# A three-part kernel (linear attention, a capacity-limited mixture of experts, a gated MLP): another order of an attention step, y in four array tiles, routing with 64-wide one-hots, and other places for pieces of the expert loop

## The chip, the cores and the metric

The kernel runs on one core of one Trainium2 chip. The metric is device microseconds (us) of one execution; lower is better. Two kernels are compared by the medians of several executions. The engines are TensorE (PE for its matmuls, PEld for its weight loads), VectorE (DVE), ScalarE (ACT), GpSimd (POOL), and SyncE (SP), which only issues DMAs here. Each engine runs its own instructions in the order written; engines meet through semaphores.

## What is computed

The reference chains three stages; the output of one is the input of the next (shapes: batch 4, 8 heads, 768 positions, head width 48; 3072 tokens of 384 values; 8 experts with 1024 hidden units; an MLP with 2048).

```python
def _attn_ref(r, k, v, w, u):
    for t in range(S):
        cur = np.einsum('bhd,bhe->bhde', u[None] * kt, vt)
        y[:, :, t] = np.einsum('bhd,bhde->bhe', rt, state + cur)
        state = wt[:, :, :, None] * state + np.einsum('bhd,bhe->bhde', kt, vt)

def _moe_ref(x, w_gate, w1, w2):
    # (token, expert) pairs by falling logit; an expert takes N // E tokens at most
    for e in range(E):
        h = np.maximum(x[mask] @ w1[e], 0.0)
        out[mask] = h @ w2[e]

def _moe2_ref(x, w_in, w_out):
    h = x @ w_in
    g = h * np.clip(h + 3.0, 0.0, 6.0) / 6.0
    return g @ w_out
```

## The kernel before

**Attention** (the function `attention`) works in 24 steps, one for each batch row `b` and chunk `c` of 128 positions, in the order n = 4c + b. A software pipeline (`pipelined`, line 43) lets every engine in its iteration m handle step m (`now`), step m-1 (`prev`) and step m-2 (`old`). The work of a step, by engine:
- DVE: scans of the decays (`fade`, L274, and `grow`, L285), `rt` (L281) and `kt` (L288) for step m; then `copy_predicated` (L295), which writes the masked scores of step m-1 over the parts of `aT` ahead of the diagonal and raises `masked`; then `total` (L302) of step m-2.
- PE: a transpose of the row of own terms (L422), the transposes of `kt` (L428), the projection `pick` (L408, heads packed and gate logits) of step m-2, the scores (L438) of step m, y from the state (L449) of step m-1, the row of own terms (L396) of step m+1, y from `aT` and `v` (L457) of step m-1, which raises `y_ready`, and the state's increment dS (L468). The scores wait for `masked` of step m-1, since they write the banks that L295 reads.
- ACT: the own terms' copy (L351), the diagonals of `aT` of step m, four activations for each half (`diagonal`, L333; the second half raises `diag_ready`), the copy of the transposed kt (L359), then the own row (L339), the copies of `pick`'s result (L374, L376), and `copy_xT` (L345) of step m-1, which waits for `y_ready`.

L295 of a step waits for `scores_ready` and `diag_ready` of that step. In each fourth step ACT and POOL also split a piece of `w_in` (L72, L78): every fp32 weight and activation of the later stages is held as a rounded part `_hi` and a remainder `_lo`, and each product is three matmuls (hi by hi, hi by lo, lo by hi; `product`, L1087).

**Routing** (DVE L834 to L945, PE L1047 to L1069) finds which expert fills first and which 384 tokens it takes: five rounds of threshold search (`cut`, `count`, `find_full`, `find_any`, `narrow`), then `candidates`, `locate`, `close`, `assign`, `name`. The ids of the tokens come from one-hots `at_q` of 128 columns (`name_q`, L938), multiplied on PE with small tables (`send_names`, L1069) and read by `take_ids` (L943 to L945). The first routing stands alone after attention; the one for expert e+1 runs inside the body of expert e.

**Experts** (`body` on each engine; e = 0 written out, 1 to 6 in a loop, 7 written out): 8 hidden tiles i of w1 and w2 (PE, with ACT L785 and DVE L989 between), the result `yT` split into hi (ACT L792) and lo (DVE L1001), then 16 tiles g of w_in and w_out, where between them stand a relu (ACT L799), the gate (DVE L1006), its rounding `act_hi` (ACT L804) and the remainder `act_lo` (POOL L735). PE computes tile g's `mid` (L1132 to L1137) and two tiles later its product with w_out. Constants (`OUT_AT_H`, `OUT_AT_G`, `NAME_AT`, `SPLIT_AT`, `SPLIT_OWN_AT` and so on) say after which i or g the pieces of routing, of splitting the next expert's weights (DVE L957) and of splitting w_out (POOL L713) are issued.

A separate block ahead of attention makes the identity matrix.

## Time and profile before

| | us |
|---|---|
| median of 3 runs | 865.16 |
| lowest, highest | 864.06, 865.38 |
| the profiled execution | 863.6 |
| its span (first to last instruction) | 861.9 |

Around the span lie 1.7 us. By engine the page gives PE 793.9 us busy (92% of the span), DVE 594.5, ACT 356.4, POOL 287.1. The span has these stages: attention until about 145 us, the first routing until 196, expert 0 until about 281, six loop bodies of 82.7 us each, and expert 7. In a row of a timeline the first number is the start, the second the length from the first start to the last modelled end; in brackets stand the idle time of the engine before it and what ended it. A matmul of 384 columns is recorded 0.33 us long while the next starts 0.17 to 0.18 us later, so where PE has waited, about 0.16 us must be added to the idle time in brackets to get what the wait cost.

### The profile page before, as it was taken

Reading aid. Unit: us, or ns where it says so; the run is one execution under the profiler, and the core shown is the slowest. Engines: PE = TensorE matmul, PEld = TensorE weight load, DVE = VectorE, ACT = ScalarE, POOL = GpSimd, SP = SyncE. Lnnn points to the kernel's source line nnn. Section 1 sums busy time; section 2 is a strip of 40 time slices with the busy share of each in tenths; the row PEclk is TensorE's granted clock in tenths of the full one; section 3 lists DMA queues with packets and bytes.
Section 4 is the critical chain, followed back from the end, with each engine's and each line's share of the span. In section 5 each row is a group of like instructions: output and inputs, shape, how many; then the busy total and the mean of one; then the engine's idle time right before and its main releaser. Section 6 shows DMA issues by size and latency. Waiting matters only on the chain.

```text
span 861.9 us, 17283 instructions
## 1 busy us (share of the span) xinstructions
PE 793.9 (92%) x6220; PEld 750.1 (87%) x6220; DVE 594.5 (69%) x1125; ACT 356.4 (41%) x783; POOL 287.1 (33%) x305
## 2 busy tenths in 40 slices
PE   5999998109999999999999999999999999999997
PEld 4999986109989999999999999999999999999996
DVE  7999997797698557665866676667667765863211
...
GB/s 299 200 246 240 213 241 56 0 125 123 74 50 115 38 0 73 100 27 0 90 93 18 21 93 86 0 49 76 76 0 49 100 52 0 49 102 51 1 1 27
DMA packets 22406, 70.13 MB, mean 81 GB/s; under 512 B 2912, under 2 KB 9312, under 8 KB 22368
## 3 DMA queue, kind: packets, MB, share of 16 engines
...
q0 software_dynamic: 3072, 9.44, 3.4%
q8 instruction: 24, 0.39, 0.2%
q14 instruction: 14, 0.11, 0.0%
...
## 4 chain that ended last, share of the span: by engine, by line
issue 40%; POOL 18%; PE 16%; DVE 5%; POOLq 2%; ACT 1%; DMA 0%; DVEq 0%; ACTq 0%
PE ps L1087 15%; POOL act_lo L735 14%; POOL out L749 3%; POOL rows L700 2%; DVE at_q L849 1%; POOLq L691 1%; DVE at_q L938 0%; DVE got L907 0%; DMA rows<-x_rows,gather_ids 0%; POOLq L734 0%; DVE cuts L846 0%; PE ps L1047 0%; ACT act_hi L804 0%; DVE w_lo L957 0%; DVE slot_add L910 0%
## 5 line engine op out<-in xcount | busy, mean ns | idle before, releaser
L735 POOL TENSOR_TENSOR act_lo<-gate,act_hi 128x384 fp32r<-128x384 f32 x128 | 146.2, 1143 | 364.5 <-ACT act_hi L804 364.0
L799 ACT ACTIVATE gate<-ps,three 128x384 f32<-128x384 f32 x128 | 74.5, 582 | 236.8 <-PE ps L1087 211.2
L1006 DVE SCALAR_TENSOR_TENSOR gate<-gate,ps 128x384 f32<-128x384 f32 x128 | 70.7, 552 | 103.1 <-ACT gate L799 100.4
L1087 PE MATMUL ps<-w_out_hi,act_hi 128*128 128x384 f32 x384 | 131.9, 344 | 6.9 <-POOL act_lo L735 6.0
L1087 PE MATMUL ps<-yT_hi,w_in_hi 128*128 128x384 f32 x384 | 132.7, 345 | 2.5 <-DVE yT_lo L1001 1.8
L1087 PE MATMUL ps<-yT_hi,w_in_lo 128*128 128x384 f32 x384 | 129.9, 338 | 0.0
L1087 PE MATMUL ps<-yT_lo,w_in_hi 128*128 128x384 f32 x384 | 129.5, 337 | 0.0
L1087 PE MATMUL ps<-w_out_hi,act_lo 128*128 128x384 f32 x384 | 128.7, 335 | 0.0
L1087 PE MATMUL ps<-w_out_lo,act_hi 128*128 128x384 f32 x384 | 128.4, 334 | 0.0
L785 ACT ACTIVATE act_hi<-ps 128x384 fp32r<-128x384 f32 x64 | 31.5, 492 | 141.8 <-PE ps L1087 140.8
L989 DVE SCALAR_TENSOR_TENSOR act_lo<-ps,act_hi 128x384 fp32r<-128x384 f32 x64 | 35.5, 555 | 77.6 <-ACT act_hi L785 77.6
L1087 PEld LDWEIGHTS ps<-w_out_hi,act_hi 128*128 128x128 f32 x384 | 72.1, 188 | 14.2 <-POOL act_lo L735 14.1
L1087 PEld LDWEIGHTS ps<-yT_hi,w_in_hi 128*128 128x128 f32 x384 | 72.1, 188 | 5.7 <-issue 4.1
L849 DVE TENSOR_TENSOR at_q<-value,cuts 128x768 bf16<-128x768 f32 x82 | 74.9, 955 | 1.4
L1087 PEld LDWEIGHTS ps<-w_out_lo,act_hi 128*128 128x128 f32 x384 | 72.1, 188 | 0.0
L1087 PEld LDWEIGHTS ps<-yT_lo,w_in_hi 128*128 128x128 f32 x384 | 72.1, 188 | 0.0
L1087 PEld LDWEIGHTS ps<-w_out_hi,act_lo 128*128 128x128 f32 x384 | 72.1, 188 | 0.0
L1087 PEld LDWEIGHTS ps<-yT_hi,w_in_lo 128*128 128x128 f32 x384 | 72.1, 188 | 0.0
L804 ACT ACTIVATE act_hi<-gate 128x384 fp32r<-128x384 f32 x128 | 66.2, 517 | 13.6 <-DVE gate L1006 13.6
L1087 PE MATMUL ps<-act_hi,w_hi 128*128 128x384 f32 x192 | 67.6, 352 | 0.0
L957 DVE TENSOR_TENSOR w_lo<-raw,w_hi 128x1024 fp32r<-128x1024 f32 x48 | 60.1, 1252 | 10.8 <-ACT w_hi L72 9.8
L72 ACT ACTIVATE w_hi<-raw 128x1024 fp32r<-128x1024 f32 x48 | 50.6, 1054 | 39.6 <-DMA raw<-in_w 39.6
...
## 6 DMA issues: line engine op xcount, KB each, us to landing
...
rows<-x_rows,gather_ids POOLq DMA_INDIRECT x24
out<-rows,scatter_ids POOLq DMA_INDIRECT x24
```

The lines of the kernel that those rows point to most:

```text
L72: act.activation(target[0][:, cols], self.raw[:, slot, :], ACT.Copy).then_inc(self.split_hi, 1)
L700: pool.indirect_dma_start(rows[:, t, :], None, x_dram, bass.IndirectOffsetOnAxis(gather_ids[:, t:t + 1], 0)).then_inc(moved, 16)
L735: pool.tensor_tensor(act[1][:, (H1 + g) % 3, :], gate[:, g % 2, :], act[0][:, (H1 + g) % 3, :].bitcast(F32), ALU.subtract).then_inc(g_lo, 1)
L749: pool.indirect_dma_start(out, bass.IndirectOffsetOnAxis(scatter_ids[:, t:t + 1], 0), rows[:, t, :], None).then_inc(moved, 16)
L785: act_.activation(act[0][:, i % 3, :], mid[i % 2], ACT.Relu).then_inc(act_hi, 1)
L799: act_.activation(gate[:, g % 2, :], mid[g % 2], ACT.Relu, bias=three[:, 0:1]).then_inc(gate_relu, 1)
L804: act_.activation(act[0][:, (H1 + g - 1) % 3, :], gate[:, (g - 1) % 2, :], ACT.Copy).then_inc(act_hi, 1)
L849: dve.tensor_tensor(above[:, half, :], value[:, half].unsqueeze(2).to_broadcast(shape), cuts[:, :].unsqueeze(1).to_broadcast(shape), ALU.i ...
L957: dve.tensor_tensor(target[1][:, cols], weights.raw[:, i % 2, :], target[0][:, cols].bitcast(F32), ALU.subtract).then_inc(expert_lo, 1)
L989: dve.scalar_tensor_tensor(act[1][:, i % 3, :], mid[i % 2], 0.0, act[0][:, i % 3, :].bitcast(F32), ALU.max, ALU.subtract).then_inc(h_lo, 1)
L1006: dve.scalar_tensor_tensor(gate[:, g % 2, :], gate[:, g % 2, :], 6.0, mid[g % 2], ALU.min, ALU.mult).then_inc(gate_ready, 1)
L1087: last = pe.matmul(out_, w, d, start=start and n == 0, stop=stop and n == len(passes) - 1)
```

## The change

- The first step's decays get a DMA of their own (`first_w`), ahead of the rest of `wrk`. The identity is made inside attention's block; the block ahead of it goes.
- y from the state goes to four 64 by 64 tiles of the array in place of two: for odd head pairs `a` the output halves are swapped (`half`), and even and odd pairs write different banks (3 and 4). `pick_gate` is permuted on the host to match, and `copy_xT` reads two banks. dS and the own row share bank 2 with the transposed kt, with waits on `ktT_copied` and `total_ready`; the own terms move to bank 4, with waits on `xT_ready` and `own_copied`.
- The order of a step changes on PE and ACT (below).
- The one-hots of `name_q` have 64 columns (`J`), `send_names` takes two tiles of tokens in a matmul (12 matmuls for 24), and `take_ids` adds the halves and writes the ids in four small operations.
- In the expert loop: `rounded` and `rest_of` order the first tile's nine matmuls so that the three that need a `_lo` activation come last; ACT issues `act_hi` of g = 0 ahead of the relu of g = 1; splits, names, gathers and the choice move by the constants; w_out's later splits on POOL are issued in halves.

PE, one full step in the steady part of attention. L438 and L444 are the scores, L449 before and L468 after are y from the state, L457 and L476 are y from `aT`. Before:

```order
L422 MATMUL attn_ps<-ident,attn_own_row 128x68
L428 MATMUL attn_ps<-ident,attn_kt 128x128 x4
L408 MATMUL attn_ps<-attn_pick_gate,attn_xT 128x104 x4
L438 MATMUL attn_ps<-attn_rt,attn_kt 128x128 x8
L449 MATMUL attn_ps<-attn_rt,attn_state 64x128 x8
L396 MATMUL attn_ps<-attn_rk,attn_u 64x128 x4
L457 MATMUL attn_ps<-attn_aT,attn_v 48x128 x8
L468 MATMUL attn_ps<-attn_v,attn_ktT 64x48 x8
```

PE, the same step after the change:

```order
L444 MATMUL attn_ps<-attn_rt,attn_kt 128x128 x8
L449 MATMUL attn_ps<-ident,attn_own_row 128x68
L454 MATMUL attn_ps<-ident,attn_kt 128x128 x4
L430 MATMUL attn_ps<-attn_pick_gate,attn_xT 128x104 x4
L468 MATMUL attn_ps<-attn_rt,attn_state 64x128 x8
L420 MATMUL attn_ps<-attn_rk,attn_u 64x128 x4
L476 MATMUL attn_ps<-attn_aT,attn_v 48x128 x8
L487 MATMUL attn_ps<-attn_v,attn_ktT 64x48 x8
```

The scores have moved from the fourth place to the first.

ACT, one full step in the same place, with the semaphores that each row waits for. Before:

```order
L351 ACTIVATE attn_own<-attn_ps 128x8 [waits attn_own_ready]
L333 ACTIVATE attn_aT<-ident,attn_own 128x128 [waits attn_y_ready,attn_own_copied]
L333 ACTIVATE attn_aT<-ident,attn_own 128x128 x3
L359 ACTIVATE attn_ktT<-attn_ps 128x512 [waits attn_dS_ready,attn_ktT_ready]
L333 ACTIVATE attn_aT<-ident,attn_own 128x128 x4
L339 ACTIVATE attn_own_row<-attn_ps 128x128 [waits attn_own_ready,attn_row_ready]
L374 ACTIVATE attn_x<-attn_ps 128x384 [waits attn_x_ready]
L376 ACTIVATE attn_logit_parts<-attn_ps 128x32
L345 ACTIVATE attn_xT<-attn_ps 128x512 [waits attn_y_ready]
```

ACT, the same step after the change:

```order
L367 ACTIVATE attn_own<-attn_ps 128x8 [waits attn_own_ready]
L372 ACTIVATE attn_ktT<-attn_ps 128x512 [waits attn_dS_ready,attn_ktT_ready]
L348 ACTIVATE attn_aT<-ident,attn_own 128x128 [waits attn_y_ready,attn_own_copied]
L348 ACTIVATE attn_aT<-ident,attn_own 128x128 x3
L354 ACTIVATE attn_own_row<-attn_ps 128x128 [waits attn_own_ready,attn_row_ready]
L387 ACTIVATE attn_x<-attn_ps 128x384 [waits attn_x_ready]
L389 ACTIVATE attn_logit_parts<-attn_ps 128x32
L361 ACTIVATE attn_xT<-attn_ps 128x2x2x128 [waits attn_y_ready]
L348 ACTIVATE attn_aT<-ident,attn_own 128x128 x4
```

The second half of the diagonals has moved from the fifth row to the last, behind the copy that waits for `y_ready`.

DVE, the first two hidden tiles of expert 0; `act_lo` is the remainder of a tile, `w_lo` a split of a weight piece, `rest` and `full_of` the verdict of a round (`find_full`). Before:

```order
L989 SCALAR_TENSOR_TENSOR act_lo<-ps,act_hi 128x384
L956 ISA
L957 TENSOR_TENSOR w_lo<-raw,w_hi 128x1024
L988 REGISTER_ALU
L989 SCALAR_TENSOR_TENSOR act_lo<-ps,act_hi 128x384
L854 ISA
L856 TENSOR_TENSOR rest<-need,ps 64x8
```

DVE, the same place after the change:

```order
L1028 SCALAR_TENSOR_TENSOR act_lo<-ps,act_hi 128x384
L1027 REGISTER_ALU
L1028 SCALAR_TENSOR_TENSOR act_lo<-ps,act_hi 128x384
L889 ISA
L891 TENSOR_TENSOR rest<-need,ps 64x8
```

The split has left the place between the two tiles.

The diff, cut to its core:

```diff
-        ktT_ps, y_ps, dS_ps, x_ps = ps[:, 2], ps[:, 3], bank(4, D), bank(5, PICK)
+        ktT_ps, dS_ps, x_ps = ps[:, 2], bank(2, D), bank(5, PICK)
+        own_row_ps = ps[:, 2].rearrange("p a t -> p (a t)")[:, PAIRS * D:PAIRS * D + PT]
+        y_ps = [ps[:, 3 + a % 2, a // 2, :] for a in range(PAIRS)]
+        y_by_bank = ps[:, 3:5, 0:PAIRS // 2, :]
+        own_ps = ps[:, 4, 2, 0:HP + H // 2]
+        own_at = ps[:, 4, 2, :].rearrange("p (g q) -> p g q", q=HP)[:, :, 0:H // 2]
...
-                    sp.dma_start(wrk[:, b, :], io["wrk"][n]).then_inc(wrk_in[b], 16)
+                    if n == 0:
+                        sp.dma_start(w[0], io["wrk"][0, :, 0:WF + 1]).then_inc(first_w, 16)
+                        sp.dma_start(wrk[:, 0, WF + 1:], io["wrk"][0, :, WF + 1:]).then_inc(wrk_in[0], 16)
+                    else:
+                        sp.dma_start(wrk[:, b, :], io["wrk"][n]).then_inc(wrk_in[b], 16)
...
-                    dve.wait_ge(wrk_in[b], 16 * (c + 1))
+                    if n == 0:
+                        dve.wait_ge(first_w, 16)
+                    else:
+                        dve.wait_ge(wrk_in[b], 16 * (c + 1))
...
-                act.activation(xT[:, b % 2], y_ps, ACT.Copy).then_inc(xT_ready, 1)
+                act.activation(xT[:, b % 2].rearrange("p (a k) t -> p k a t", k=2), y_by_bank, ACT.Copy).then_inc(xT_ready, 1)
...
                     n, b, c = now
                     act.wait_ge(own_ready, n + 1)
                     act.activation(own[:, b % 2].rearrange("p a h -> p (a h)").rearrange("p (g q) -> p g q", g=2),
-                                   own_at[c == CHUNKS - 1], ACT.Copy).then_inc(own_copied, 1)
-                    act.wait_ge(own_copied, n + 1)
-                    wait(act, y_ready, n - 1)
-                    diagonal(b, 0)
+                                   own_at, ACT.Copy).then_inc(own_copied, 1)
                     if c < CHUNKS - 1:
                         act.wait_ge(ktT_ready, n + 1)
                         wait(act, dS_ready, n - 1)
                         act.activation(ktT[:, b % 2], ktT_ps, ACT.Copy).then_inc(ktT_copied, 1)
-                    diagonal(b, 1).then_inc(diag_ready, 1)
-                    if b == 1:
-                        weights.hi(act, weights.w_in, bass.ds(c * PART, PART), c % 2, c // 2)
+                    act.wait_ge(own_copied, n + 1)
+                    wait(act, y_ready, n - 1)
+                    diagonal(b, 0)
                 if now and n + 1 < STEPS:
                     copy_row(n + 1)
...
                 if prev and now:
                     copy_xT(*prev)
+                if now:
+                    n, b, c = now
+                    diagonal(b, 1).then_inc(diag_ready, 1)
+                    if b == 1:
+                        weights.hi(act, weights.w_in, bass.ds(c * PART, PART), c % 2, c // 2)
...
+            def half(a, h):
+
+                return HP * (h if a % 2 == 0 else 1 - h)
...
+                wait(pe, ktT_copied, min(n, STEPS - B))
...
-                    pe.wait_ge(row_copied, n + 1)
-
-                    wait(pe, own_copied, n)
-                    if c < CHUNKS - 1:
-                        wait(pe, x_copied, n - 2)
-                    pe.transpose(own_ps[c == CHUNKS - 1], own_row[0:HP + H // 2, :], ident[0:HP + H // 2, 0:HP + H // 2]
-                                 ).then_inc(own_ready, 1)
                     pe.wait_ge(qk_ready, n + 1)
-                    if c < CHUNKS - 1:
-                        wait(pe, ktT_copied, n)
-                        for a in range(PAIRS):
-                            last = pe.transpose(ktT_ps[:, a, :], kt[:, b, a, :], ident[:, :])
-                        last.then_inc(ktT_ready, 1)
-                if old and (now or not prev):
-                    pick(old[0], old[1], now)
-                if now:
-                    n, b, c = now
                     wait(pe, masked, n)
                     for a in range(PAIRS):
                         for h in range(2):
                             part = slice(HP * h, HP * h + HP)
                             last = pe.matmul(ps[:, h, a, :], kt[part, b, a, :], rt[part, b, a, :], start=True, stop=True)
                     last.then_inc(scores_ready, 1)
-                    if n == 0:
-                        send_row(1)
+                    pe.wait_ge(row_copied, n + 1)
+                    wait(pe, own_copied, n)
+                    wait(pe, xT_ready, n - 1)
+                    pe.transpose(own_ps, own_row[0:HP + H // 2, :], ident[0:HP + H // 2, 0:HP + H // 2]).then_inc(own_ready, 1)
+                    if c < CHUNKS - 1:
+                        wait(pe, ktT_copied, n)
+                        wait(pe, total_ready, n - 1)
+                        for a in range(PAIRS):
+                            last = pe.transpose(ktT_ps[:, a, :], kt[:, b, a, :], ident[:, :])
+                        last.then_inc(ktT_ready, 1)
+                if old and (now or not prev):
+                    pick(old[0], old[1])
+                if now and now[0] == 0:
+                    send_row(1)
...
+                    pe.wait_ge(own_copied, min(n + 2, STEPS))
                     for a in range(PAIRS):
                         for h in range(2):
                             part = slice(HP * h, HP * h + HP)
-                            pe.matmul(y_ps[part, a, :], state[part, b, a, :], rt[part, b, a, :],
-                                      start=(a == 0), stop=True, skip_group_check=True)
+                            pe.matmul(y_ps[a][half(a, h):half(a, h) + HP, :], state[part, b, a, :], rt[part, b, a, :],
+                                      start=(a < 2), stop=True, skip_group_check=True)
                     if now:
                         send_row(n + 2)
                     pe.wait_ge(masked, n + 1)
                     pe.wait_ge(v_in[b], 16 * (c + 1))
...
-OUT_AT_H, OUT_AT_G = (3, 5, 6), (0, 1, 4)
-LOCATE_AT, NAME_AT, GATHER_AT, CHOOSE_AT, XT_AT = 4, 9, 9, 12, 16
+OUT_AT_H, OUT_AT_G = (5, 6, 7), (1, 3, 5)
+OUT_HALVES = {g + half: (len(OUT_AT_H) + i, half) for i, g in enumerate(OUT_AT_G) for half in range(2)}
+LOCATE_AT, NAME_AT, GATHER_AT, CHOOSE_AT, XT_AT = 4, 8, 8, 11, 16
 SPLIT_AT = (8, 10, 12, 14)
-SPLIT_OWN_AT = (0, 2)
+SPLIT_OWN_AT = (2, 4)
...
-                    q = MIDS * e + H1 + g
-                    if g < H2:
-                        act_.wait_ge(mid_ready, q + 1)
-                        if g >= 2:
-                            act_.wait_ge(g_lo, H2 * e + g - 1)
-                        act_.activation(gate[:, g % 2, :], mid[g % 2], ACT.Relu, bias=three[:, 0:1]).then_inc(gate_relu, 1)
+                    if g < H2 and g != 1:
+                        relu(g)
                     if g > 0:
                         act_.wait_ge(gate_ready, H2 * e + g)
                         if g > 3:
                             act_.wait_ge(g_used, (H2 - 1) * e + g - 3)
                         act_.activation(act[0][:, (H1 + g - 1) % 3, :], gate[:, (g - 1) % 2, :], ACT.Copy).then_inc(act_hi, 1)
+                    if g == 1:
+                        relu(1)
...
-                shape = [128, TILES // 2, 128]
-                dve.tensor_tensor(at_q[:, tiles, :], to_127[:, :].unsqueeze(1).to_broadcast(shape),
+                shape = [128, TILES // 2, J]
+                dve.tensor_tensor(at_q[:, tiles, :], to_63[:, :].unsqueeze(1).to_broadcast(shape),
...
-                link(dve.tensor_copy(ids_f[:, :], ids_ps[:, ET:2 * ET]))
-                dve.scalar_tensor_tensor(gather_ids[:, :], ids_ps[:, 0:ET], float(PT), ids_f[:, :], ALU.mult, ALU.add)
-                dve.scalar_tensor_tensor(new_ids[:, :], ids_ps[:, 0:ET], float(PT), ids_f[:, :],
-                                         ALU.mult, ALU.add).then_inc(ids_ready, 1)
+                link(dve.tensor_copy(odd_ids[:, :], ids_ps[J:2 * J, 2 * GROUPS:4 * GROUPS]))
+                link(dve.tensor_tensor(all_ids[:, :, :, :].rearrange("q c t h -> q (c t h)"), ids_ps[0:J, 0:2 * GROUPS],
+                                       odd_ids[:, :], ALU.add))
+                for ids in (gather_ids, new_ids):
+                    for h in range(2):
+                        last = dve.scalar_tensor_tensor(ids[h * J:h * J + J, :], all_ids[:, 0, :, h], float(PT),
+                                                        all_ids[:, 1, :, h], ALU.mult, ALU.add)
+                last.then_inc(ids_ready, 1)
...
-                    if g == NAME_AT - 2:
+                    if g == NAME_AT - 1:
                         name_q(e, 0)
-                    if g == NAME_AT - 1:
                         name_q(e, 1)
...
+            def rounded(out_, weight, data, start):
+
+                pe.matmul(out_, weight[0], data[0], start=start, stop=False)
+                pe.matmul(out_, weight[1], data[0], start=False, stop=False)
+
+            def rest_of(out_, weight, data, stop):
+
+                return pe.matmul(out_, weight[0], data[1], start=False, stop=stop)
...
+                        if i == 0:
+                            for k in range(KC):
+                                pe.wait_ge(xT_hi, 3 * e + k + 1)
+                                pe.wait_ge(expert_lo, 2 * LOADS * e + k + 1)
+                                rounded(mid[0], *of_w1(k), k == 0)
+                            for k in range(KC):
                                 pe.wait_ge(xT_lo, 3 * e + k + 1)
...
+    pick_gate[:, :, 1::2] = pick_gate[::-1, :, 1::2].copy()
```

## Rows read from the trace of the kernel before

**Rows 1.** Windows: busy us (count) of PE, PEld, DVE, ACT, POOL; clock; DMA

```profile
21.93:123.52 101.59, 101.51 (x1527) 91.93 (x1526) 96.74 (x127) 83.61 (x256) 43.87 (x47) 1.00 0.65 225
148.00:151.20 3.20, 0.76 (x4) 0.38 (x4) 2.23 (x14) 0.49 (x1) 0.00 (x0) 1.00 0.34 123
151.20:196.01 44.81, 8.15 (x101) 5.61 (x101) 36.73 (x92) 4.15 (x5) 4.08 (x4) 0.50 0.19 64
```

**Rows 2.** Timeline of PE over one attention step: start, us, what

```profile
71.21 0.28 PE L422 MATMUL attn_ps<-ident,attn_own_row 68*128 68x68 f32 x1
71.33 0.60 PE L428 MATMUL attn_ps<-ident,attn_kt 128*128 128x128 f32 x4
71.81 1.11 PE L408 MATMUL attn_ps<-attn_pick_gate,attn_xT 128*128 128x104 f32 x8
72.84 1.16 PE L438 MATMUL attn_ps<-attn_rt,attn_kt 64*128 64x128 f32 x16
73.94 1.09 PE L449 MATMUL attn_ps<-attn_rt,attn_state 64*64 64x128 f32 x16
74.96 0.66 PE L396 MATMUL attn_ps<-attn_rk,attn_u 128*64 128x128 f32 x8
75.44 1.04 PE L457 MATMUL attn_ps<-attn_aT,attn_v 128*48 128x128 f32 x16
76.32 0.62 PE L468 MATMUL attn_ps<-attn_v,attn_ktT 128*64 128x48 f32 x16
...
78.50 1.16 PE L438 MATMUL attn_ps<-attn_rt,attn_kt 64*128 64x128 f32 x16
```

**Rows 3.** Timeline of ACT and of DVE in the same step

```profile
72.92 0.58 ACT L359 ACTIVATE attn_ktT<-attn_ps 128x512 f32<-128x512 f32 x1
73.40 1.27 ACT L333 ACTIVATE attn_aT<-ident,attn_own 128x128 f32<-128x128 f32 x4
76.53 0.60 ACT L345 ACTIVATE attn_xT<-attn_ps 128x512 f32<-128x512 f32 x1
...
75.40 1.36 DVE L295 COPY_PREDICATED attn_aT<-attn_earlier,attn_ps 128x1024 f32<-128x1024 int32 x1
76.98 0.36 DVE L302 TENSOR_TENSOR attn_total<-attn_ps,attn_state 128x192 f32<-128x192 f32 x1 [0.22 <-PE attn_ps L468]
```

**Rows 4.** Timeline of PE at the start and the end of attention

```profile
8.40 1.12 PE L396 MATMUL attn_ps<-attn_rk,attn_u 128*64 128x128 f32 x8 [8.40 <-DMA attn_pick_gate<-in_pick_gate]
...
11.44 2.08 PE L438 MATMUL attn_ps<-attn_rt,attn_kt 64*128 64x128 f32 x16
...
15.93 0.38 PE L438 MATMUL attn_ps<-attn_rt,attn_kt 64*128 64x128 f32 x2 [0.25 <-DVE attn_aT L295]
...
139.81 1.16 PE L438 MATMUL attn_ps<-attn_rt,attn_kt 64*128 64x128 f32 x16
...
144.81 1.08 PE L457 MATMUL attn_ps<-attn_aT,attn_v 128*48 128x128 f32 x16
```

**Rows 5.** Timeline of DVE at the end of the first routing

```profile
181.97 3.43 DVE L938 TENSOR_TENSOR at_q<-to,q_f 128x1536 bf16<-128x1536 bf16 x2
```

**Rows 6.** Timeline of PE: where it waited in the expert bodies

```profile
250.33 0.44 PE L1087 MATMUL ps<-yT_hi,w_in_hi 128*128 128x384 f32 x1 [0.79 <-DVE gate L1006]
310.52 0.42 PE L1087 MATMUL ps<-yT_hi,w_in_hi 128*128 128x384 f32 x1 [0.22 <-DVE yT_lo L1001]
316.06 0.44 PE L1087 MATMUL ps<-w_out_hi,act_hi 128*128 128x384 f32 x1 [0.21 <-POOL act_lo L735]
340.27 0.76 PE L1069 MATMUL ps<-names,at_q 128*128 128x6 bf16 x24
361.82 0.44 PE L1087 MATMUL ps<-w_out_hi,act_hi 128*128 128x384 f32 x1 [0.39 <-POOL act_lo L735]
370.61 0.18 PE L1055 MATMUL ps<-full,ones 128*128 128x1 bf16 x1 [0.28 <-DVE full L858]
809.39 0.44 PE L1087 MATMUL ps<-w_out_hi,act_hi 128*128 128x384 f32 x1 [0.58 <-POOL act_lo L735]
```

112 lines of the change are left out of this document (66 added, 46 removed).

## The prediction

> **What bounds the kernel now.** I read the windows first, then the timeline of one attention step engine by engine, then the edges of attention, then the places where PE waited in the expert bodies. The first window runs from the scores of step 2 to those of step 20: 18 steps in 101.59 us, 5.64 us each, PE marked busy in all of it, DVE in 96.74 of it [rows 1]. In the timeline of PE the groups of a step follow each other without a wait, and the next step's scores start 5.66 us after the last ones (72.84 to 78.50) [rows 2]. DVE has 0.22 us a step in which it waits for PE's dS [rows 3]. So attention is bound by PE's own work, with DVE close behind. In the experts PE is bound too; what can be had there are its few waits [rows 6].
>
> **The order of an attention step.** This is the part that decides. Follow the semaphores after the change. The scores of step m+1 wait for `masked` of step m. That is the predicated copy on DVE, which waits for `diag_ready` of step m. The second half of the diagonals, which raises it, now stands behind `copy_xT` of step m-1 on ACT, and ACT issues in order. `copy_xT` waits for `y_ready` of step m-1, and y from `aT` of step m-1 is issued by PE in the same iteration as the scores of step m, and behind them. That closes a circle: scores, then nearly all of PE's step, then ACT, then DVE, then the next scores. Before, the diagonals needed only the own terms (PE's first group); they ended at 74.67 and the copy started at 75.40, so they were never late [rows 3].
>
> What one turn of the circle costs, from the starts of successive groups [rows 2]: scores 1.10 us (73.94 - 72.84, the change of array tiling at its end included), own terms 0.12, transposes of kt 0.48, `pick` 1.03, y from the state 0.60 (below), own row 0.48, y from `aT` to its end 1.04: together 4.85. Then ACT starts `copy_xT` 0.05 us after y's end (76.48 to 76.53); the next activation starts about 0.50 after that (after the 0.58 us copy it took 0.48); four diagonals 1.27; about 0.03 to DVE; the predicated copy 1.36; 0.05 back to PE [rows 3]. That is 3.26. One turn takes 8.11 us, against 5.66: 2.45 us more a step. PE's dS, DVE's scans (all of DVE's step is under 5.4 us) and POOL's work lie beside it and cost nothing.
>
> y from the state: eight matmuls are 16 records, two at a time in two diagonal tiles, in 1.02 us (73.94 to 74.96) [rows 2], some 0.11 us a pair and 0.2 for the change of tiling. With four tiles at once half of the steps of 0.11 go: 1.02 - 4 x 0.11 = 0.58, and I take 0.60. That four run at once no row shows. The upper bound is no gain, 1.02; a loss is excluded, since only the halves of odd pairs move. I take 0.60 because y from `aT` shows two column tiles over the same rows with different data (16 records in 76.32 - 75.44 = 0.88) and the scores show two row tiles: both directions are there.
>
> That row also answers a rule. The Trainium skill ("TensorE: Matmul & The Clock Gate", Part 3, The mechanism) says that weight loads overlap with running matmuls only where the row groups differ. By it even and odd pairs, on the same rows, would take turns, and y would stay at 1.02. The y from `aT` just quoted runs two at a time on one row group, which speaks against it.
>
> Summed over attention:
> - Steps 2 to 19, 18 turns: 18 x 2.45 = +44.1.
> - The last three turns have no transposes of kt: 8.11 - 0.48 = 7.63. The stretch from 123.52 [rows 1] to 139.81 [rows 4] is 16.29 us for three, 5.43 each. +6.6.
> - Turn 1 has no `pick`: 8.11 - 1.03 = 7.08, against 6.00 (15.93 [rows 4] to 21.93 [rows 1]). +1.1.
> - After the last scores: now the last y from `aT` starts 5.00 us later (139.81 to 144.81) [rows 4]; then it needs the whole turn, 7.63. +2.6. DVE's early choice of experts stands ahead of the last predicated copy and fits into its wait.
> - The start. Without the block of its own, and with the first DMA a little ahead, PE's first group, which waits for `pick_gate`'s DMA at 8.40 [rows 4], comes about 1.0 us sooner (a bound from below of 0; the queue is the same). The scores of step 0 then start at about 8.5 and not 11.44, but PE and the circle at the slow clock (scores 2.0, transposes 1.0, own row 1.1 behind the kt copy of 0.6, then 0.3 + 1.27 + 1.36 and handoffs) put step 1's at about 16.5 against 15.93 [rows 4]. +0.6, between -1.5 and +2.
>
> Together +55.0 us.
>
> **The routing that stands alone.** Two one-hot operations take 3.43 us at 128 columns [rows 5]; half as wide, 1.7 less 0.1: -1.6. The names of six groups and not three, one more linked operation and two more small ones in `take_ids` give back about 0.6. -1.0. The first tile's `rounded` part starts before the remainders of xT: -0.3. Sum -1.3.
>
> **The expert bodies.** To the bracketed idle times 0.16 us is to be added [rows 6].
> - The verdict of a round comes late in tile 1 because a split stands ahead of it on DVE: 0.28 + 0.16 = 0.44. With the split two tiles on, where DVE has room (there was one after tile 2 before), this goes. Seven bodies: -3.1.
> - Between the hidden tiles and w_in PE waits 0.22 + 0.16 for the remainder of y; at the first w_out tile 0.21 + 0.16 for POOL. The new order of the nine matmuls removes the first and the earlier `act_hi` most of the second, but DVE still has a cut ahead of the first gate, so the two give 0.41 together, not 0.75. Seven bodies -2.9. The last body has no cut: 0.38 + 0.74 = -1.1.
> - Names: 24 small matmuls in 0.76 us; half of them less, 0.3. -2.1.
> - Behind the transposes PE waits 0.39 for a remainder that POOL makes while DVE works off a cut and a split; the cut now stands one tile earlier. Half of it, -1.3.
> - In body 0 a late gate costs 0.79 + 0.16, behind DVE operations that POOL's long splits slow; halves and other places: -1.0.
>
> Sum -11.5, between -5 and -16; the lower end if POOL's gathers meet the same tiles as before and `take_ids`, which is longer, delays a gate.
>
> **Sum.** 863.6 + 55.0 - 1.3 - 11.5 = 905.8 for the profiled execution. The median of before lies 1.6 above its profiled execution, so 907.4; I say 907.
>
> **The rivals.**
> - *Pairs stay pairs.* The y from the state remains at 1.02. Then a turn is 8.53, and 0.42 x 23 = 9.7 us more: 917. For it: no row has four tiles; against it: y from `aT`. This is also what the rule above gives.
> - *The clock falls.* Each turn leaves PE without work from dS's end to the next scores: dS ends 5.4 us into a turn of 8.11, so 2.7 us. Before, the clock was at 1.00 (2.4 GHz) through attention, and went to 0.50 (1.2 GHz) at 151.2, behind 3.20 us in which PE was busy for 0.76 [rows 1]. If it fell in the turns, PE's 4.85 would near the pace of step 0 (scores 2.0 for 1.1) and grow by about 4.3: held down half of the time, +2.1 x 22 = 47, so 954. Against it: PE is busy for two thirds of a turn, and between 8.40 and 15.93, with waits between the groups, it came up (scores 2.08 long in step 0, 1.16 later) [rows 2, 4]. The Trainium skill (the same page, Part 1) has the clock halved by idleness and released by activity; the rows bear that out, and they leave open what two thirds would do.
> - *Faster than before.* The circle is not what binds: ACT gets past `copy_xT` in time. The place is ACT's queue between the row's copy and the diagonals. It decides at one point: with 3.26 us behind y's end, PE's stretch from the scores to that end must be under 2.4 us for the step to stay at 5.66, and it is 4.85 with every group in its written place. If the circle fell away, DVE would set about 5.36 us a step: -0.3 x 22 = -6.6, and 865.2 - 6.6 - 12.8 = 846. Only a misread order would give this.
> - *The bodies turn worse.* The gathers, the longer `take_ids` and two ACT splits in the last hidden tiles of body 0 cost as much as they free: -11.5 becomes 0, 919.
>
> **How the numbers follow.** Main case (four tiles, clock up, the bodies gain 5 to 16) 0.63, 900 to 915; pairs 0.14; bodies without gain 0.08; clock 0.09; no circle 0.05; 0.01 for a tie. The range 896 to 922 takes in the first three (about 0.85, less the tails) and leaves out the clock and the other side. Within 0.2% is about what a measurement can tell from no change. Faster 0.05, same 0.01, slower 0.94.
>
> **What would show it.** In the timeline of the changed kernel the scores come every 8.1 us; the predicated copy waits about 2.7 us a step for ACT's diagonals, and the diagonals follow `copy_xT` at once; PE's scores wait for the predicated copy. y from the state takes 0.6 us to the next group (pairs: 1.0). The clock stays at 1.00 until after attention. Attention ends near 200 us. In a loop body the waits for `full`, `yT_lo` and the first `act_lo` are gone and its length is near 81.4 us, not 82.7. I am wrong if the scores come every 5.4 us, if the clock column shows 0.50 inside attention, or if the diagonals start before y's end.

## The result: slower, and by more than forecast

The changed kernel takes 935.85 us (median of 4 runs, 933.97 to 938.06), the kernel before 864.61 us in the same comparison (863.86 to 865.38). The ratio is 1.0829, with a 95% interval of 1.0815 to 1.0843. The forecast was 907, with a range of 896 to 922: the direction was right, the size was not. The profiled execution of the changed kernel took 933.97 us, with a span of 932.2; that of before had a span of 861.9. All stage times below are from these two.

The page of the changed kernel: the span, PE's busy tenths and the clock in 40 slices, and two groups of attention (busy us, mean ns | idle before, releaser).

```profile
span 932.2 us, 17153 instructions
...
PE   5676766666219989999999999999999999999997
...
PEclk8888888897559989999999999999999999999999
...
L444 PE MATMUL attn_ps<-attn_rt,attn_kt 64*128 64x128 f32 x384 | 33.4, 320 | 68.1 <-DVE attn_aT L309 68.1
L309 DVE COPY_PREDICATED attn_aT<-attn_earlier,attn_ps 128x1024 f32<-128x1024 int32 x24 | 31.2, 1299 | 92.2 <-ACT attn_aT L348 92.2
```

Two things are new. PE waits 68.1 us before the scores (L444) for DVE's predicated copy (L309), and that copy waits 92.2 us for ACT's diagonals (L348). And the clock's row stands at 8, not 9, through the first eight slices, up to 186 us; attention ends near 230.

Now one attention turn on PE; compare [rows 2]. Start, us, what, and in brackets the idle time before it and who ended it.

```profile
119.15 1.16 PE L444 MATMUL attn_ps<-attn_rt,attn_kt 64*128 64x128 f32 x16 [2.90 <-DVE attn_aT L309]
120.24 0.28 PE L449 MATMUL attn_ps<-ident,attn_own_row 68*128 68x68 f32 x1
120.36 0.60 PE L454 MATMUL attn_ps<-ident,attn_kt 128*128 128x128 f32 x4
120.80 1.04 PE L430 MATMUL attn_ps<-attn_pick_gate,attn_xT 128*128 128x104 f32 x8
121.77 0.67 PE L468 MATMUL attn_ps<-attn_rt,attn_state 64*64 64x128 f32 x16
122.36 0.66 PE L420 MATMUL attn_ps<-attn_rk,attn_u 128*64 128x128 f32 x8
122.85 1.04 PE L476 MATMUL attn_ps<-attn_aT,attn_v 128*48 128x128 f32 x16
...
127.24 0.38 PE L444 MATMUL attn_ps<-attn_rt,attn_kt 64*128 64x128 f32 x2 [2.90 <-DVE attn_aT L309]
```

The same turn on ACT and DVE; compare [rows 3].

```profile
123.95 0.60 ACT L361 ACTIVATE attn_xT<-attn_ps 128x512 f32<-128x512 f32 x1
124.44 1.26 ACT L348 ACTIVATE attn_aT<-ident,attn_own 128x128 f32<-128x128 f32 x4
...
125.81 1.29 DVE L309 COPY_PREDICATED attn_aT<-attn_earlier,attn_ps 128x1024 f32<-128x1024 int32 x1 [2.77 <-ACT attn_aT L348]
```

This is the forecast circle, link by link: scores at 119.15, y from `aT` at 122.85, the xT copy at 123.95, the diagonals at 124.44, the predicated copy at 125.81, the next scores at 127.24. The turn is 8.09 us; forecast were 8.11. y from the state takes 0.59 us to the next group (121.77 to 122.36); forecast were 0.60, and before it was 1.02. But this is a turn at the full clock, and most are not. The turn before it on PE:

```profile
109.47 1.16 PE L444 MATMUL attn_ps<-attn_rt,attn_kt 64*128 64x128 f32 x16 [2.90 <-DVE attn_aT L309]
110.56 0.28 PE L449 MATMUL attn_ps<-ident,attn_own_row 68*128 68x68 f32 x1
110.67 0.99 PE L454 MATMUL attn_ps<-ident,attn_kt 128*128 128x128 f32 x4
111.45 1.88 PE L430 MATMUL attn_ps<-attn_pick_gate,attn_xT 128*128 128x104 f32 x8
113.26 1.08 PE L468 MATMUL attn_ps<-attn_rt,attn_state 64*64 64x128 f32 x16
114.27 0.66 PE L420 MATMUL attn_ps<-attn_rk,attn_u 128*64 128x128 f32 x8
```

`pick` takes 1.88 us, not 1.04, and y from the state 1.08, not 0.67; the turn takes 9.68 us. The windows show the clock over the stages: the window, its length, busy us of PE, PEld, DVE, ACT and POOL, the mean granted clock, DMA. Compare [rows 1].

```profile
15.98:25.98 10.00, 7.06 (x77) 6.06 (x78) 5.03 (x8) 4.92 (x13) 1.82 (x2) 0.67 0.33 124
25.98:191.76 165.78, 113.49 (x1531) 102.44 (x1531) 94.76 (x127) 83.79 (x256) 43.92 (x46) 0.87 0.41 140
191.76:219.12 27.36, 17.74 (x211) 15.21 (x212) 15.53 (x21) 12.83 (x40) 6.10 (x6) 0.77 0.17 63
...
119.15:127.24 8.09, 5.20 (x85) 4.70 (x86) 5.25 (x8) 4.45 (x14) 1.79 (x2) 1.00 0.61 221
109.47:119.15 9.68, 6.78 (x85) 6.10 (x86) 5.25 (x8) 4.45 (x14) 1.78 (x2) 0.82 0.37 124
...
110.80:114.10 3.30, 3.30 (x29) 3.00 (x27) 2.52 (x4) 1.94 (x6) 0.67 (x1) 0.50 0.04 14
```

The 18 turns from scores 2 to scores 20 take 165.78 us, 9.21 each. At 8.09 they would take 145.6; the other 20.2 us are the clock. It goes back and forth between 1.00 and 0.50 inside the turns: in the turn of 9.68 us it stands at 0.50 from about 110.8 to 114.1, while PE works without a pause, and is back at 1.00 for its last groups. Six of the 18 turns take 8.1 us, eleven take 9.6 to 9.7, and the first takes 10.93.

Where the 70.3 us between the two spans lie (starts of the named groups, after less before):

| stage | forecast | measured |
|---|---|---|
| to scores 1 | +0.6 | +0.05 (15.98 for 15.93) |
| turn 1 | +1.1 | +4.0 (10.00 for 6.00) |
| turns 2 to 19 | +44.1 | +64.2 (165.78 for 101.59) |
| last three turns | +6.6 | +11.1 (27.36 for 16.29) |
| last scores to last y from `aT` | +2.6 | +4.1 (9.11 for 5.00) |
| routing alone | -1.3 | -0.7 |
| bodies | -11.5 | -12.4 |

### The profile page after: what moved, and what is told of

It reads as the page before. It is cut to its first block, busy times and chain, and to the rows that moved or that the text cites. A ratio compares the mean times of both kernels' runs of the same rounds, so it can differ in the third digit from the quotient of the medians.

```text
span 932.2 us, 17153 instructions
## 1 busy us (share of the span) xinstructions
PE 804.6 (86%) x6124; PEld 766.2 (82%) x6124; DVE 577.0 (62%) x1149; ACT 357.3 (38%) x783; POOL 269.0 (29%) x308
## 4 chain that ended last, share of the span: by engine, by line
PE 65%; DVE 5%; issue 2%; POOL 1%; ACT 0%; DMA 0%; POOLq 0%; DVEq 0%; ACTq 0%
PE ps L1126 61%; DVE at_q L884 1%; PE ps L1085 1%; PE ps L1117 1%; PE ps L1131 1%; PE ps L1132 1%; PE ps L1136 1%; DVE gate L1045 0%; DVE at_q L973 0%; DVE cuts L881 0%; ACT yT_hi L823 0%; DMA rows<-x_rows,gather_ids 0%; POOL out L780 0%; PE ps L1107 0%; DVE slot_add L945 0%
## 5 line engine op out<-in xcount | busy, mean ns | idle before, releaser
L766 POOL TENSOR_TENSOR act_lo<-gate,act_hi 128x384 fp32r<-128x384 f32 x128 | 134.7, 1055 | 365.2 <-ACT act_hi L837 365.1
L1126 PE MATMUL ps<-yT_hi,w_in_hi 128*128 128x384 f32 x360 | 123.9, 344 | 1.0
L1126 PE MATMUL ps<-yT_hi,w_in_lo 128*128 128x384 f32 x360 | 121.9, 339 | 0.0
L1126 PE MATMUL ps<-yT_lo,w_in_hi 128*128 128x384 f32 x360 | 121.6, 338 | 0.0
L444 PE MATMUL attn_ps<-attn_rt,attn_kt 64*128 64x128 f32 x384 | 33.4, 320 | 68.1 <-DVE attn_aT L309 68.1
L309 DVE COPY_PREDICATED attn_aT<-attn_earlier,attn_ps 128x1024 f32<-128x1024 int32 x24 | 31.2, 1299 | 92.2 <-ACT attn_aT L348 92.2
L444 PEld LDWEIGHTS attn_ps<-attn_rt,attn_kt 64*128 64x128 f32 x384 | 28.3, 217 | 71.2 <-issue 71.2
L1126 PEld LDWEIGHTS ps<-yT_hi,w_in_hi 128*128 128x128 f32 x360 | 68.0, 189 | 2.2 <-DVE gate L1045 1.7
L1126 PEld LDWEIGHTS ps<-yT_lo,w_in_hi 128*128 128x128 f32 x360 | 68.1, 189 | 0.0
L1126 PEld LDWEIGHTS ps<-yT_hi,w_in_lo 128*128 128x128 f32 x360 | 68.0, 189 | 0.0
```

Of the source, the lines that this page charges most:

```text
L309: dve.copy_predicated(aT[:, b % 2].rearrange("p h a t -> p (h a) t"), earlier[:, :].unsqueeze(1).to_broadcast([PT, H, PT]), ps[:, 0:2].rea ...
L444: last = pe.matmul(ps[:, h, a, :], kt[part, b, a, :], rt[part, b, a, :], start=True, stop=True)
L766: pool.tensor_tensor(act[1][:, (H1 + g) % 3, :], gate[:, g % 2, :], act[0][:, (H1 + g) % 3, :].bitcast(F32), ALU.subtract).then_inc(g_lo, 1)
L1126: last = pe.matmul(out_, w, d, start=start and n == 0, stop=stop and n == len(passes) - 1)
```

## The experiments

Three questions were open. Is the clock's fall really caused by PE's waits in the circle, and is it worth all of the missing 28 us? Is the circle made by the place of the diagonals on ACT alone, or also by PE's new order and the shared banks? What is the rest of the change worth alone? Each run is compared with the kernel before on the same chip, whose median is 864.6 to 865.3 us in all of them.

| run | median us | ratio to before (95%) | mean turn 2 to 19 |
|---|---|---|---|
| changed kernel | 935.85 | 1.083 (1.082 to 1.084) | 9.21 |
| e1 eleven fillers | 908.67 | 1.051 (1.049 to 1.053) | 8.14 |
| e5 five fillers | 922.91 | 1.067 (1.063 to 1.071) | 8.79 |
| e6 fillers, pairs | 916.25 | 1.060 (1.058 to 1.062) | 8.56 |
| e3 before, diagonals late | 905.96 | 1.048 (1.046 to 1.050) | 7.27 |
| e2 diagonals early | 861.11 | 0.996 (0.994 to 0.997) | 6.20 |
| e7 own terms first | 852.88 | 0.987 (0.985 to 0.989) | 5.72 |
| e8 and names later | 855.39 | 0.989 (0.988 to 0.991) | 5.72 |
| e9 own terms in bank 5 | 847.78 | 0.980 (0.978 to 0.983) | 5.47 |
| e10 and start as changed | 845.45 | 0.978 (0.977 to 0.980) | 5.47 |
| e4 rest alone | 850.90 | 0.984 (0.982 to 0.986) | 5.64 |
| e11 rest, split early | 852.66 | 0.986 (0.983 to 0.989) | 5.64 |

**Is it the clock?** More work for PE, and nothing else, behind dS:

```diff
                 if old and prev and not now:
                     pick(old[0], old[1])
+                if old and prev and now:
+                    pe.wait_ge(x_copied, old[0] + 1)
+                    for _ in range(11):
+                        pe.matmul(ps[:, 5, 3, 32:128], ident[:, :], ident[:, 0:96], start=True, stop=True)
```

> The changed kernel plus eleven matmuls of 128x96 a step on PE, behind dS, whose results nobody reads (nothing else is changed). One of them should take about 0.25 us, as pick's four of 104 columns take 1.03 us, so they fill 2.7 of the 2.9 us that PE waits in a turn. Theory (the clock falls because PE is idle in each turn): the granted clock stays at 1.00 from scores 2 to scores 20, the turn stays near 8.1 to 8.3 us instead of the mean of 9.2, and the time falls from 936 to between 903 and 912, although PE has more to do. Rival 1 (the chip holds the clock down because PE does too much, or for a reason outside the kernel): the clock alternates as before or is lower, turns of 9.2 us or more, time 936 or more. Rival 2 (the slow turns have another cause, and the clock only goes along): clock up, but the mean turn still above 9 us, 936.

```profile
79.26 2.69 PE L493 MATMUL attn_ps<-ident 128*128 128x96 f32 x22
82.27 0.94 PE L444 MATMUL attn_ps<-attn_rt,attn_kt 64*128 64x128 f32 x12 [0.32 <-DVE attn_aT L309]
...
25.00:190.00 165.00, 157.91 (x2157) 145.80 (x2157) 109.00 (x145) 93.97 (x288) 49.18 (x51) 1.00 0.44 150
```

The fillers take 2.69 us a turn, 0.32 us of the wait is left, the window's clock is 1.00, and the turn is 8.12 to 8.16 us from turn 2 on. The time falls by 27 us to 908.67, although PE does 22 times 2.69 us, 59 us, of work more. So the idle time in the turn is what lowers the clock, and the clock explains the miss: 908.67 against a forecast of 907 that left it out. Both rivals fall.

With `range(5)` for `range(11)`:

> As the run with eleven unread matmuls a step, but with five: about 1.25 us of the 2.9 us that PE waits in a turn is filled, some 1.7 us stay idle. If the clock depends on how long PE stands in each turn, it falls less often than in the changed kernel and more often than never: between 1 and 8 stretches at 0.50 in attention, mean turn 8.15 to 8.9 us, time 911 to 928. If only a single long wait matters (each of 1.7 us is shorter than what brought it down), the clock stays at 1.00 and the time is 907 to 910. If any filling is useless until the wait is gone, 930 to 936.

```profile
107.28 1.16 PE L444 MATMUL attn_ps<-attn_rt,attn_kt 64*128 64x128 f32 x16 [1.61 <-DVE attn_aT L309]
...
25.00:190.00 165.00, 134.17 (x1765) 122.25 (x1767) 100.03 (x133) 86.49 (x265) 46.04 (x48) 0.91 0.43 147
```

With 1.61 us of wait left the clock still falls, but less often: eight of the 18 turns take over 9.4 us, where twelve do in the changed kernel. The clock is 0.91 in the window, the mean turn 8.79, the time 922.91 us. It is a matter of degree. The four runs of this kernel spread from 918.96 to 926.13, while those of the kernel that stays at 1.00 lie within 2.2 us.

**Who makes the circle?** First ACT's order alone is turned back in the changed kernel:

```diff
                                    own_at, ACT.Copy).then_inc(own_copied, 1)
+                    act.wait_ge(own_copied, n + 1)
+                    wait(act, y_ready, n - 1)
+                    diagonal(b, 0)
...
-                    act.wait_ge(own_copied, n + 1)
-                    wait(act, y_ready, n - 1)
-                    diagonal(b, 0)
+                    diagonal(b, 1).then_inc(diag_ready, 1)
+                    if b == 1:
+                        weights.hi(act, weights.w_in, bass.ds(c * PART, PART), c % 2, c // 2)
...
-                if now:
-                    n, b, c = now
-                    diagonal(b, 1).then_inc(diag_ready, 1)
-                    if b == 1:
-                        weights.hi(act, weights.w_in, bass.ds(c * PART, PART), c % 2, c // 2)
```

> The changed kernel with only ACT's order of a step as in the kernel before: own terms, first diagonals, kt copy, second diagonals (and the split of w_in), row, x, xT. Four tiles, banks and PE's order stay as changed. Theory (the circle through the xT copy is what costs the time): the diagonals no longer wait for y, the circle left is scores, own terms, ACT's diagonals, the predicated copy, scores: 1.10 + 0.12 + about 3.3 + 1.4 = 6.0 us, or PE's own 5.3, so the turn is between 5.4 and 6.2 us, the clock stays at 1.00, and the time is between 850 and 866. Rival (PE's order or the shared banks make most of the loss): a turn stays over 7 us and the time over 885.

```profile
90.72 1.16 PE L442 MATMUL attn_ps<-attn_rt,attn_kt 64*128 64x128 f32 x16 [0.53 <-DVE attn_aT L309]
...
94.35 0.66 PE L418 MATMUL attn_ps<-attn_rk,attn_u 128*64 128x128 f32 x8 [0.35 <-ACT attn_ktT L375]
...
25.00:125.00 100.00, 85.45 (x1379) 76.13 (x1378) 86.28 (x114) 73.02 (x231) 38.55 (x40) 1.00 0.61 207
```

861.11 us: that order alone costs 75 us. The turn is 6.14 us, 6.40 in each fourth, where the split of w_in stands on ACT. It is the smaller circle that was expected (6.0), with two short waits on PE, and the clock stays at 1.00 in this window. Even so its turn is longer than before the change (5.64).

Then the mirror image, the kernel before with only its second diagonals (and the split) behind the xT copy:

```diff
-                    diagonal(b, 1).then_inc(diag_ready, 1)
-                    if b == 1:
-                        weights.hi(act, weights.w_in, bass.ds(c * PART, PART), c % 2, c // 2)
...
+                if now:
+                    n, b, c = now
+                    diagonal(b, 1).then_inc(diag_ready, 1)
+                    if b == 1:
+                        weights.hi(act, weights.w_in, bass.ds(c * PART, PART), c % 2, c // 2)
```

> The kernel before with only ACT's order of a step as changed: the second diagonals (and the split of w_in) behind the xT copy; PE's order, pairs of tiles and banks as before. Theory: the same circle, but shorter, since fewer groups of PE lie between the scores and the end of y: 1.10 + 1.02 + 0.48 + 1.04 + 3.26 = 6.9 us a turn; PE idles about 1.2 us of it. If that idle is short enough to leave the clock at 1.00, the time is 864.6 + 22 x 1.25 = 892 (887 to 897). If any idle time in every turn brings the clock down for a part of the turns, it is 5 to 20 us more, 897 to 912, with 0.50 in the clock's row inside attention. Rival (the place of the diagonals is harmless by itself): 865.

```profile
60.91 1.11 PE L410 MATMUL attn_ps<-attn_pick_gate,attn_xT 128*128 128x104 f32 x8 [0.86 <-issue]
62.26 1.16 PE L440 MATMUL attn_ps<-attn_rt,attn_kt 64*128 64x128 f32 x16 [0.23 <-DVE attn_aT L295]
...
82.71 1.33 PE L410 MATMUL attn_ps<-attn_pick_gate,attn_xT 128*128 128x104 f32 x8 [1.82 <-issue]
...
25.00:190.00 165.00, 133.02 (x1841) 116.25 (x1841) 118.65 (x166) 99.50 (x312) 50.59 (x52) 0.97 0.45 153
```

905.96 us, 41 more than before, where 892 was expected and 897 to 912 allowed if the clock came down. The undisturbed turn is 6.95 us (expected 6.9). From the starts of the scores, the first two turns cost 4.8 us more than before (one of them 9.22, with the clock at 0.50 for a part), turns 2 to 19 cost 29.2 and the last three 6.1. Of the 29.2, 18 x 1.31 = 23.6 are the circle. The split of w_in makes each fourth turn 7.60, 2.6 in all; behind the diagonals it holds up ACT's next step, and I had not priced it. The other 3 are the clock, which fell twice (turns of 8.28 and 8.52 us). Both falls came behind a turn with the split in it, where PE stands 1.8 us ahead of `pick` (the row at 82.71) and not 0.86; two more such turns had no fall, and none came in these 18 turns behind the usual 0.86 and 0.23. So the late diagonals are harmful with the old order of PE too. In the changed kernel, with its scores ahead of everything and its shorter y from the state, the circle is 1.1 us longer still.

**Do four tiles run at once, and why?** The run e1 with the halves of odd pairs not swapped:

```diff
-                return HP * (h if a % 2 == 0 else 1 - h)
+                return HP * h
...
-    pick_gate[:, :, 1::2] = pick_gate[::-1, :, 1::2].copy()
```

> The run with eleven unread matmuls a step, with y of odd pairs put back into the diagonal tiles (the halves not swapped, the host's order of pick_gate neither); banks and order stay as changed. Theory (four 64x64 tiles run at once, and the swapped halves are what makes them): y from the state takes 1.02 us to the next group and not 0.59, each turn 0.42 us more, 8.13 becomes 8.55, the time 908.7 + 22 x 0.42 = 918 (915 to 920). Rival (the two banks, not the swapped halves, shorten it): 0.59 stays, the time 907 to 910.

```profile
80.02 1.09 PE L468 MATMUL attn_ps<-attn_rt,attn_state 64*64 64x128 f32 x16
81.04 0.66 PE L420 MATMUL attn_ps<-attn_rk,attn_u 128*64 128x128 f32 x8
```

1.02 us instead of 0.60, a turn of 8.56 instead of 8.14, a time of 916.25 us (expected 918), with the banks unchanged. The swapped halves alone are worth 0.42 us a turn. The weight loads (PEld) of y from the state, in the kernel before and then in the changed one, halve as well:

```profile
73.93 0.85 PEld L449 LDWEIGHTS attn_ps<-attn_rt,attn_state 64*64 64x64 f32 x16
...
121.76 0.42 PEld L468 LDWEIGHTS attn_ps<-attn_rt,attn_state 64*64 64x64 f32 x16
```

The Trainium skill ("TensorE: Matmul & The Clock Gate", Part 3, The mechanism) lets weight loads overlap with running matmuls only where the row groups differ. By that sentence alone 1.02 would have stayed, since each row group serves two of the four tiles. The trace disagrees.

**What was in the way of PE?** On e2, PE's own terms go back ahead of the scores:

```diff
                     if n == 0:
                         send_row(0)
+                    pe.wait_ge(row_copied, n + 1)
+                    wait(pe, own_copied, n)
+                    wait(pe, xT_ready, n - 1)
+                    pe.transpose(own_ps, ...).then_inc(own_ready, 1)
                     pe.wait_ge(qk_ready, n + 1)
```

> The run with ACT's order of before, and on PE the own terms put back ahead of the scores; four tiles and banks as changed. In that run the turn of 6.14 us is a circle: scores and own terms on PE, then ACT's own copy to the predicated copy's end 4.6 us. With the own terms first, nothing between them and the next own terms needs the predicated copy. Theory: the turn falls to what PE needs (0.12 + 1.10 + 0.48 + 1.03 + 0.60 + 0.48 + 1.04 + 0.45 = 5.3 us) or DVE (5.4), so 5.3 to 5.6 us; 20 turns by 0.7: 861 - 14 = 847 (843 to 851). Rival (another wait takes its place, such as the row behind the kt copy in the shared bank 2): a turn of 5.8 us or more, 853 and up.

```profile
62.50 0.62 PE L485 MATMUL attn_ps<-attn_v,attn_ktT 128*64 128x48 f32 x16
63.47 0.25 PE L440 MATMUL attn_ps<-ident,attn_own_row 68*128 68x68 f32 x1 [0.34 <-ACT attn_xT L361]
```

852.88 us: 8 less than e2, not 14, and outside the 843 to 851 expected. The rival held in part, though not at the row that it named: the turn is 5.65 us, because the own terms share bank 4 with y and wait for ACT's xT copy. The next run moves them to bank 5:

```diff
-        own_ps = ps[:, 4, 2, 0:HP + H // 2]
+        x_bank = ps[:, 5].rearrange("p a t -> p (a t)")
+        own_ps = x_bank[:, PAIRS * PICK:PAIRS * PICK + HP + H // 2]
...
+                pe.wait_ge(own_copied, min(n + 3, STEPS))
...
-                    wait(pe, xT_ready, n - 1)
+                    wait(pe, x_copied, n - 2)
...
-                    pe.wait_ge(own_copied, min(n + 2, STEPS))
```

> The run with the own terms first, and their PSUM columns moved from bank 4, which y uses, back to bank 5 behind pick's (in all steps), with the waits that go with it. In the run before, the turn was 5.65 us and not 5.3 to 5.4: PE's own terms start at 63.466, some 0.5 us after dS, because they wait for ACT's xT copy (62.724 for 0.597 us) out of the shared bank. Theory: in bank 5 they need only ACT's x copy, which ends 0.6 us sooner, so the turn falls to DVE's own sum of about 5.4 us: 20 turns by 0.25, 852.9 - 5 = 848 (846 to 850). Rival (the turn of 5.65 is DVE's or ACT's own work, whatever the bank): 5.6 us or more and 851 to 854.

```profile
61.41 0.28 PE L442 MATMUL attn_ps<-ident,attn_own_row 68*128 68x68 f32 x1
```

DVE in the same turn:

```profile
60.15 1.36 DVE L310 COPY_PREDICATED attn_aT<-attn_earlier,attn_ps 128x1024 f32<-128x1024 int32 x1
...
65.60 1.34 DVE L310 COPY_PREDICATED attn_aT<-attn_earlier,attn_ps 128x1024 f32<-128x1024 int32 x1
```

The wait ahead of the own terms is gone, and DVE now runs from one predicated copy to the next in 5.45 us without a gap: it is the bound. The mean turn is 5.47 us (5.72 in e7), the time 847.78 us, as expected. The last run of this row puts only step 0's own terms behind the scores:

```diff
-                    pe.wait_ge(row_copied, n + 1)
...
+                    if n > 0:
+                        send_own(n)
...
                     last.then_inc(scores_ready, 1)
+                    if n == 0:
+                        send_own(0)
```

> The run before this, but in step 0 alone the own terms behind the scores as in the changed kernel. In the run with the own terms first the scores of step 0 start at 10.34 us instead of 8.1, and those of step 1 at 16.80 instead of 15.19 (the run with the own terms second). Theory: this gives back 1 to 2 us at the start, 847. Rival (step 1 is set by the clock and by ACT's and DVE's chain anyway): 0, 848.

The scores of step 0 start at 8.10 us instead of 10.19, those of step 1 at 15.20 instead of 16.64. The median is 845.45, 2.3 less, but the runs of the two overlap (844.34 to 847.17, 845.16 to 848.76). The traces show 1.4 us at scores 1, within the 1 to 2 expected. Another 1.0 lies in body 0, which this row doesn't touch: there the clock fell for a part in e9 and not in this run (see body 0, below). This version beats both kernels, by 2.2% the one before.

**The rest of the change.** The attention of before with the tables, routing and bodies of the changed kernel:

> The attention of the kernel before with the routing and the expert bodies of the changed kernel: what the change does behind attention, alone. From the two traces: routing -0.7, body 0 +2.0, bodies 1 to 6 six times -2.1, last body -1.7, together -13.0, so 851.6 (850 to 853). If the bodies gain only because attention ends in another state (loads that landed earlier in the longer attention), the gain is smaller and the time is above 855.

850.90 us (expected 851.6), and later bodies of 80.6 us as in the changed kernel. So what stands behind attention is worth 14 us by itself, and it is worth as much behind the one attention as behind the other. In it, one placing is undone:

```diff
-SPLIT_OWN_AT = (2, 4)
+SPLIT_OWN_AT = (0, 2)
```

> The run with the attention of before and the bodies of the changed kernel, with one thing undone in the bodies: the two splits of its own weights behind hidden tiles 0 and 2, as before the change, not 2 and 4. Theory (the split behind tile 0 makes the first verdicts late): 0.28 + 0.16 = 0.44 us a body over seven bodies, 3.1 us more than 850.9, so 854.0 (853.5 to 854.5), and PE's wait for DVE's full is back with twelve occurrences. Rival (the saving in the bodies comes from elsewhere, and this wait would be hidden by another): 851.

PE's waits for a verdict (us in total, times, longest), first in the rest alone:

```profile
PE ps L1074 <- DVE full L874: 3.2, 5, 0.6
```

With the split early:

```profile
PE ps L1074 <- DVE full L874: 4.9, 11, 0.6
...
370.40 0.18 PE L1074 MATMUL ps<-full,ones 128*128 128x1 bf16 x1 [0.28 <-DVE full L874]
```

From transposes to transposes the later bodies take 81.05 us instead of 80.60: 0.45 each, where 0.44 was expected. The wait occurs 11 times, where twelve were expected, and 5 times without the early split. The median, 852.66, misses the 853.5 to 854.5 and lies between the theory and the rival's 851. Its runs go from 850.87 to 855.54; the two shorter ones had a mean clock of 0.970, the two longer ones 0.967, as all four of e4 had. The trace is the better witness here. On e7, the names, gathers and choice go one hidden tile back:

```diff
-LOCATE_AT, NAME_AT, GATHER_AT, CHOOSE_AT, XT_AT = 4, 8, 8, 11, 16
+LOCATE_AT, NAME_AT, GATHER_AT, CHOOSE_AT, XT_AT = 4, 9, 9, 12, 16
```

> The run with the own terms first, and in every expert body the names, the gathers and the next choice one hidden tile later (9, 9 and 12 for 8, 8 and 11, as before the change). Theory: body 0 loses the two waits of 3.1 to 3.7 us in which PE waits for DVE's at_q, which runs late because POOL's halves of the w_out split stretch DVE's operations beside them; bodies 1 to 6 do not change. 3 us less than the run with the own terms first, about 844. Rival (the gathers one tile later meet the end of the body, or w_out's halves stretch something else): 0 to +3 us.

```profile
442.15 0.45 PE L1124 MATMUL ps<-w_out_hi,act_hi 128*128 128x384 f32 x1 [0.36 <-POOL act_lo L764]
```

A miss, and a useful one. Body 0 does get shorter, by 1.7 us (83.79 to 82.08), but each of the next six gets longer by 0.95 (80.58 to 81.53), and the median is 2.5 us worse. The wait behind the transposes is back: 0.36 us here, 0.39 in [rows 6]. It makes 0.6 of the 0.95: the group behind the transposes starts 1.50 us into the body (440.65 to 442.15), and 0.90 in e7. Of the 1.7 us in body 0 a part is the clock, which stood at 0.50 there for a while in e7 and not in e8 (see body 0, below).

## Why the forecast was wrong

**What bounds, and the circle: right.** The order of the semaphores gave the circle, and the durations of [rows 2, 3] gave its length: 8.11 forecast, 8.09 in the trace and 8.14 in e1, where the clock is out of play. e2 and e3 showed that the place of the diagonals makes it.

**y from the state: right.** 0.60 forecast, 0.59 measured; e6 gives the 0.42 us back by unswapping the halves alone.

**The start: right to 0.6 us.** Scores 0 at 8.09 (forecast 8.5), scores 1 at 15.98 (16.5).

**The clock: this step failed.** The text saw it: PE would stand 2.7 us in each turn, and the price of a fall was put at 2.1 us a turn, 954 in all. Then it argued that a PE that is busy for two thirds of a turn keeps its clock, from the start of attention, where the clock had come up in spite of waits, and gave the fall 0.09 and the main case a clock of 1.00. The waits of the turn were in fact enough. The clock neither stayed up nor stayed down: it alternated, at a mean of 0.87, and the price was 1.12 us a turn (9.21 less 8.09).

The price of a clock that is down throughout had been about right: 0.87 means 0.50 for 26% of the time, and 26% of the 4.3 us by which PE's work was to grow is 1.1. Its share of the time was not: half in the rival, none in the main case. Over attention 29 us lie above the forecast: 20.2 in turns 2 to 19, 2.9 in turn 1, 4.5 in the last three turns and 1.5 behind them, at mean clocks of 0.87, 0.67, 0.77 and 0.77 in turn. e1 takes 27.2 us off the time by keeping PE busy. The row at the start could not carry the argument: it showed that the clock can rise between waits, not that it stays up under them. No case of the clock had been priced between 907 and 954, so the range ended at 922, just above the other rivals (917 and 919) and under the case that came.

**Routing: -0.7 for -1.3.** Too small to have been tested apart.

**The bodies: the sum right by luck.** -12.4 for -11.5, but two misses of over 4 us cancel in it. Each of bodies 1 to 6 was to gain 1.3 us (0.44 + 0.41 + 0.30 + 0.19) and gained 2.1. Body 0 was to gain the same and 1.0 of its own, 2.3, and became longer by 2.0. The last body gained 1.7 for 1.1.

In the later bodies the forecast let a part of three waits stand. The four waits of such a body in [rows 6], 0.39, 0.28, 0.22 and 0.21 with 0.16 each, are 1.74 us, and it counted 1.04 of them as saved. In the changed kernel none of the four is among PE's waits from 400 us on. The names gave 0.22 (0.62 to 0.40 until the next group), forecast 0.30. The verdict is 0.45 us a body (e11; forecast 0.44). For the wait behind the transposes the forecast took half of 0.39, and for the places of names and gathers nothing; e8 shows 0.95 a body for names, gathers and choice together, and no run divides it by these three.

In body 0 it failed twice. The first place is the names' small matmuls, two rows of PE in the changed kernel:

```profile
335.82 0.31 PE L1107 MATMUL ps<-names,at_q 128*128 128x24 bf16 x6 [1.80 <-DVE at_q L973]
337.48 0.34 PE L1107 MATMUL ps<-names,at_q 128*128 128x24 bf16 x6 [1.36 <-DVE at_q L973]
```

The second is the same step as in attention: behind these waits the clock falls. From 336.0 to 342.8 the window row has it at 0.50:

```profile
336.00:342.80 6.80, 5.44 (x28) 5.35 (x25) 4.62 (x10) 2.05 (x3) 1.41 (x2) 0.50 0.43 160
```

The matmuls of 384 columns start every 0.32 us in it, and not every 0.17. The same two waits stand in e7, e9 and e10, with another length of the fall: body 0 takes 85.56 us here, 83.79 in e7 and 83.95 in e9, where the fall is shorter, and 82.96 in e10, where there is none. By that the fall is worth up to 2.6 us here; without it body 0 would have become some 0.6 us shorter, where 2.3 was forecast, and not 2.0 longer.

The names come one tile sooner, and DVE is not ready: in body 0 its operations beside POOL's are long. DVE's `at_t` and `at_q`, and POOL beside the second, start and us:

```profile
332.20 1.34 DVE L965 TENSOR_TENSOR at_t<-group_no,t_f 128x144 f32<-128x144 f32 x1
...
334.81 2.62 DVE L973 TENSOR_TENSOR at_q<-to,q_f 128x768 bf16<-128x768 bf16 x2
...
335.53 1.08 POOL L766 TENSOR_TENSOR act_lo<-gate,act_hi 128x384 fp32r<-128x384 f32 x1 [2.15 <-ACT act_hi L837]
```

In the body behind it `at_t` takes 0.31 us and the two `at_q` 1.82. Here POOL's half of the w_out split lies beside `at_t` (332.10 for 1.28 us), but what lies beside `at_q` is `act_lo`, which every tile has. That an operation on POOL stretches one on DVE is read from their lying side by side; no run took the split away. e8 shows only that the earlier names cause the wait.
